# Attention scores and state pass on four 64x64 quarters of the matrix array, in a linear-attention and mixture kernel

## The reference, cut to what matters

```python
# attention: batch 8, heads 8, sequence 576, head width 64, all fp32
scores = scale * np.matmul(q, k.transpose(0, 1, 3, 2))
gamma = 1.0 - 2.0 ** (-5.0 - np.arange(H, dtype=np.float32))
Dmat = np.where(rel >= 0, gamma[:, None, None] ** rel[None, :, :], 0.0)
ret = scores * Dmat[None, :, :, :]
x = np.matmul(ret, v)
...
# then, on 4608 tokens x 512: a soft mixture of 8 experts with 32 slots, and
# a, b = x @ w1, x @ w2 ; out = (a * b) @ w3 @ w_out
```

## Time and profile before

| what | value |
|---|---|
| median of 3 runs (lowest, highest) | 434.02 us (432.9, 434.08) |
| the profiled execution's own time | 434.21 us |
| its span, first to last instruction | 432.4 us |
| granted TensorE clock, mean | 0.995 of 2.4 GHz |
| PE busy | 402.9 us, 93% |
| DVE, ACT, POOL busy | 172.8, 137.3, 165.4 us |
| bytes moved by DMA | 103.57 MB, 240 GB/s on average |

### The profile page before, as it was taken

The page is one execution under the profiler, slowest core; times in us unless marked ns, Lnnn a source line. Parts: engine busy times, 40 slices in busy tenths (PEclk is TensorE's granted clock), DMA queues, the critical chain, the costliest instruction groups (busy, mean ns, idle before and its releaser), DMA issues.

```text
span 432.4 us, 8735 instructions
## 1 busy us (share of the span) xinstructions
PE 402.9 (93%) x3375; PEld 298.1 (69%) x3375; DVE 172.8 (40%) x276; ACT 137.3 (32%) x278; POOL 165.4 (38%) x154
## 2 busy tenths in 40 slices
PE   2899998999999999899999999959989999998897
PEld 2888686878688778746454544448768888787775
DVE  1444364545454545335003100289852344423550
ACT  0224222232233223342233321413254444323442
POOL 2212212122111221074444442078865366544560
PEclk9999999999999999999999999989999999999999
DMA  7986979799969898988979999042222444344432
GB/s 251 314 296 223 332 272 386 236 306 305 385 234 314 306 344 278 343 278 258 330 227 342 386 387 405 7 91 100 93 93 103 171 174 157 116 172 172 172 124 97
DMA packets 50551, 103.57 MB, mean 240 GB/s; under 512 B 4128, under 2 KB 8416, under 8 KB 50528
## 3 DMA queue, kind: packets, MB, share of 16 engines
q1 hardware_dynamic: 50528, 103.26, 68.3%
HBM read 92.92 MB, written 10.32 MB: 239 GB/s over the span
## 4 chain that ended last, share of the span: by engine, by line
PE 73%; DMA 12%; DVE 4%; POOL 3%; SPq 3%; issue 3%; ACT 2%; ACTq 0%; DVEq 0%; POOLq 0%
PE psum L948 14%; PE psum L762 12%; PE psum L618 8%; PE psum L645 8%; PE psum L777 7%; PE psum L635 7%; DMA c_sb<-c_rows 6%; DMA pkg_sb<-in_tiles 5%; PE psum L684 4%; PE psum L916 4%; PE psum L670 3%; PE psum L719 3%; PE psum L695 2%; SPq L510 2%; POOL feat L590 2%
## 5 line engine op out<-in xcount | busy, mean ns | idle before, releaser
L546 POOL TENSOR_TENSOR pkg_sb<-pkg_sb,const_sb 128x512 f32<-128x512 f32 x36 | 37.5, 1042 | 137.8 <-DMA pkg_sb<-in_tiles 137.8
L590 POOL TENSOR_TENSOR feat<-c_sb 128x512 f32<-128x512 f32 x45 | 62.6, 1413 | 45.7 <-DMA c_sb<-c_rows 29.5
L1136 DVE TENSOR_TENSOR weights_t<-psum,const_sb 128x512 f32<-128x512 f32 x72 | 49.2, 690 | 74.2 <-PE psum L645 40.1
L948 PE MATMUL psum<-m_hi,feat_hi 128*128 128x512 f32 x144 | 56.6, 393 | 5.0 <-ACT out_sb L1117 3.4
L948 PE MATMUL psum<-m_hi,feat_lo 128*128 128x512 f32 x144 | 56.1, 390 | 0.0
L948 PE MATMUL psum<-m_lo,feat_hi 128*128 128x512 f32 x144 | 56.0, 389 | 0.0
L618 PE MATMUL psum<-pkg_sb 64*128 64x128 f32 x576 | 43.7, 293 | 11.6 <-DMA pkg_sb<-in_tiles 11.4
L394 DVE TENSOR_TENSOR feat_lo<-feat,feat_hi 128x512 fp32r<-128x512 f32 x32 | 28.4, 888 | 60.3 <-ACT feat_hi L1085 58.3
L618 PEld LDWEIGHTS psum<-pkg_sb 64*128 64x128 f32 x576 | 36.7, 195 | 18.1 <-issue 13.6
L969 ACT COPY state_sb<-psum 64x256 f32<-64x256 f32 x64 | 23.5, 367 | 80.1 <-PE psum L670 79.3
L1085 ACT CAST feat_hi<-feat 128x512 fp32r<-128x512 f32 x45 | 27.7, 624 | 55.6 <-POOL feat L590 55.6
(11 more groups left out here) (126 smaller groups left out, 540.3 us busy)
## 6 DMA issues: line engine op xcount, KB each, us to landing
pkg_sb<-in_tiles SPq DMA_DIRECT2D x72, 256.0 KB, 5.7
pkg_sb<-in_tiles SPq DMA_DIRECT2D x36, 512.0 KB, 5.6
unit_a<-in_moe_w SPq DMA_DIRECT2D x10, 1024.0 KB, 8.3
c_sb<-c_rows SPq DMA_DIRECT2D x36, 256.0 KB
out<-out_sb SPq DMA_DIRECT2D x36, 256.0 KB, 7.0
unit_a<-in_moe_w SPq DMA_DIRECT2D x14, 512.0 KB, 6.9
fold_raw<-in_moe_fold SPq DMA_DIRECT2D x12, 512.0 KB, 7.2
unit_x<-in_moe_w SPq DMA_DIRECT2D x6, 1024.0 KB, 6.8
```

Source lines behind the costliest of these rows:

```text
L546: nc.gpsimd.tensor_tensor(v_nat(t).rearrange("p (h d) -> p h d", h=HEADS), v_nat(t).rearrange("p (h d) -> p h d", h=HEADS), decay.unsqueez ...
L590: nc.gpsimd.tensor_tensor(feat[:, k, :], c_sb[:, s, x, :], c_sb[:, s, y, :], ALU.mult).then_inc(feat_ready, 1)
L948: last = mm(psum[:, OUT + b, :], x, y, start=(at == 0 and m == 0), stop=(at == 4 and m == 2))
L1136: tt(weights_t[:, u % 3, :].rearrange("p (i n) -> p i n", i=4), psum[:, u % 3, :].rearrange("p (i n) -> p i n", i=4), const_sb[:, m:m + P] ...
```

## The change

The attention's layout changes; what is computed stays the same, except that a quarter of the scores, which the mask would set to zero, isn't computed.

- Scores: each head's multiplication is cut in two by keys. One half of the keys (64) goes to PSUM partitions 0 to 63, the other to 64 to 127, so that with even and odd heads on the two halves of the input partitions there are four 64x64 quarters of the array. In the half with the later keys only the later 64 queries are computed, 64 columns in place of 128. For heads 4 to 7 the halves are swapped (the host swaps k and v and the masks too). 16 multiplications for a tile in place of 8. Even heads write bank 0, odd heads bank 1; with two banks in place of three, `scores` waits for both masks of the tile before it.
- State pass: 8 multiplications 64x64 against 128 queries in place of 4 with 128x128; `state_sb` holds states alone, without zeros, and ACT copies it in one instruction of 128 partitions x 256. It is issued right behind `scores`, ahead of the first transposes and of `through_scores`, in tile 4 too.
- Outputs lie in two banks, one for even and one for odd heads, half a bank each.
- The masked scores have four buffers in place of three; both masks of a tile wait for the outputs of the tile two before it.
- In tile 4 the state is summed over all 128 partitions; POOL sets the first half of k to zero (one more instruction of 128x512 for a group).
- The mask constants grow by 256 columns and two more are added: `const_sb` gets 0.13 MB more.
- The loops over groups 1 to 3 are written out on every engine.

```diff
-        OUT_T, STATE, X_NAT, LOGITS, MISC = 3, 4, 5, 6, 7
+        OUT_T, STATE, X_NAT, LOGITS, MISC = 2, 4, 5, 6, 7
...
             def scale_v(g, t):
                 pool.wait_ge(natural_loaded[t % 3], (g * 3 + (t // 3 + 1)) * 16)
+                if t == SEAM:
+
+                    k = k_nat(t).rearrange("p (b n) -> p b n", b=2)
+                    second = const_sb[:, C_SEAM:C_SEAM + 2].unsqueeze(2).to_broadcast([P, 2, D // 2])
+                    nc.gpsimd.tensor_tensor(k, k, second, ALU.mult)
...
-                    pe.wait_ge(masked, g * (2 * TILES) + (2 * t - 1))
+                first = is_first(g) and t == 0
+                if not first:
+
+                    pe.wait_ge(masked, g * (2 * TILES) + 2 * t)
                 for a in range(PAIRS):
                     for odd in range(2):
-                        last = mm(psum[:, (2 * t + odd) % 3, P * a:P * (a + 1)], k_t(t)[HD * odd:HD * (odd + 1), a, :],
-                                  q_t(t)[HD * odd:HD * (odd + 1), a, :], start=True, stop=True)
...
+                        rows = slice(HD * odd, HD * (odd + 1))
+                        for half in range(2):
+
+                            later = half == (0 if a >= 2 else 1)
+                            lo = HD if later and not first else 0
+                            last = mm(psum[HD * half:HD * (half + 1), odd, P * a + lo:P * (a + 1)],
+                                      k_t(t)[rows, a, HD * half:HD * (half + 1)], q_t(t)[rows, a, lo:P],
+                                      start=True, stop=True)
+                            if a == PAIRS - 1:
+                                last.then_inc(scores_ready[odd], 1)
...
+            def through_state(g, t):
+
+
+                pe.wait_ge(x_t_ready, g * TILES + t)
+                pe.wait_ge(state_copied, g * STATES + t)
+                n = P // 2 if t == SEAM else P
+                for a in range(PAIRS):
+                    for odd in range(2):
+                        rows = slice(HD * odd, HD * (odd + 1))
+                        mm(out_of(a, odd, n), state_sb[rows, (t - 1) % 2, a, :], q_t(t)[rows, a, 0:n],
+                           start=(a < 2), stop=True, skip_group_check=True)
...
                 for t in range(TILES):
                     if t < TILES - 1:
                         scores(g, t + 1)
+                    if t > 0:
+                        through_state(g, t)
                     for turned in TURNS[t][:-1]:
                         turn_x(g, turned)
-                    outputs(g, t)
+                    through_scores(g, t)
...
-            with pe.Fori(1, GROUPS) as g:
+            for g in range(1, GROUPS):
                 group(g)
...
-                for r in (0, HD):
-                    copy(state_sb[r:r + HD, t % 2, :, r:r + HD], bank[r:r + HD, :, :]).then_inc(state_copied, 1)
+                copy(state_sb[:, t % 2, :, :].rearrange("p a n -> p (a n)"),
+                     psum[:, STATE, 0:PAIRS * HD]).then_inc(state_copied, 1)
...
-                    if not (is_first(g) and u < 3):
-
-                        dve.wait_ge(out_ready, g * TILES + (t - 1 + hf))
+                    if not (is_first(g) and t < 2):
+
+                        dve.wait_ge(out_ready, g * TILES + (t - 1))
```

More of the change, by code:

```diff
@@ L224, in build @@
         natural_loaded = [sem(f"natural_loaded{i}") for i in range(3)]
[L225 removed]
         v_ready = sem("v_ready")
[L227 removed]
+        scores_ready = [sem(f"scores_ready{i}") for i in range(2)]
         masked = sem("masked")
@@ new lines, in through_scores @@
+            def through_scores(g, t):
+                if t == 0 and not is_first(g):
+                    pe.wait_ge(x_t_ready, g * TILES)
+                pe.wait_ge(masked, g * (2 * TILES) + (2 * t + 2))
+                pe.wait_ge(v_ready, g * TILES + (t + 1))
+                for half in range(2):
+                    for odd in range(2):
+                        for a in (2 * half, 2 * half + 1):
+                            h = 2 * a + odd
+                            last = mm(out_of(a, odd), v_nat(t)[:, HD * h:HD * (h + 1)],
+                                      weights_t[:, (2 * t + odd) % 4, P * a:P * (a + 1)],
+                                      start=(t == 0 and a < 2), stop=True, skip_group_check=True)
@@ L851, in _ @@
             for k in range(4):
-                last = mm(psum[:, MISC, SLOTS * k:SLOTS * (k + 1)], group_sum[:, 0, P * k:P * (k + 1)], fold_rows,
-                          start=True, stop=True)
+                for odd in range(2):
+                    at = HD * PAIRS * odd + HD * k
+                    last = mm(psum[HD * odd:HD * (odd + 1), MISC, SLOTS * k:SLOTS * (k + 1)],
+                              group_sum[:, 0, at:at + HD], fold_rows, start=True, stop=True)
             last.then_inc(slot_in_turned, 1)
@@ L1009, in group @@
                         exp_combine(g - 1)
-            act.wait_ge(state_zeroed, 1)
             group(0)
-            with act.Fori(1, GROUPS) as g:
+            for g in range(1, GROUPS):
                 group(g)
@@ L1200, in _ @@
             group(0)
-            with dve.Fori(1, GROUPS) as g:
+            for g in range(1, GROUPS):
                 group(g)
```

111 lines of the change are left out of this document (48 added, 63 removed).

## The result

The changed kernel takes 424.25 us (median of 4 runs, 421.86 to 425.01) against 433.85 for the kernel before beside it (4 runs, 432.9 to 434.08): a ratio of 0.9772, 95% interval 0.9747 to 0.9798. The gain is 9.6 us; 21.7 were forecast. The profiled execution of the changed kernel took 424.09, its span is 422.3 and its clock 0.987.

A forecast was written before the change was run, and what follows sets the result against it. Attention was taken as TensorE-bound with the DMA queue close behind. Groups 1 to 3 save 3 x (7.7 - 2.5) = 15.6 us, group 0 6.1, together 21.7: 434.21 to 412.5 us, own range 408 to 416, whole range 404 to 422.

The forecast's parts named there:

- (a): Scores: four quarters run at once, each at its own pace, 0.68 us of passes; 0.88 kept as a rival.
- lock step: Rival, chance 0.27: each set of four score passes waits for its longest, left-out quarter worth no time; 417.5 us.
- (b): State pass: 16 passes on four quarters, 0.44 us in place of 0.88, one change of array shape gone.
- only two quarters at a time: Rival, chance 0.07: scores and state pass run only two quarters at once; slower, 440 us.
- (c): Tiles 4 and 5: cheaper seam state pass and tile 5 scores and state pass, less one shape change; 1.9 us saved.
- (d): Tile 8, without scores: shorter state pass and the 0.41 us wait for x_t gone; 0.8 us saved.
- (e): Tile 0: two score blocks alone, 0.25 us saved on each, 0.5 together.
- (f): Group 0: ACT's table load runs ahead, so the first state pass starts at about 16.1, not 17.40; 1.2 us saved.
- (g): Costed at nothing: single state copy, masks, score and output banks, POOL's extra multiplication, written-out loops, small multiplications after the attention.
- the queue's share: Gain lost to DMA waits for q: 2.5 of 7.7 us a group in groups 1 to 3, 2.3 in group 0.
- The queue takes more: Rival, chance 0.13: requests stay at 302 to 317 GB/s, groups last 43 us as now; 422 us.

The follow-up runs named there:

- e10: The kernel before, with the 12 requests for first-unit weights issued behind the last tile's; 431.77 us.
- e7: The changed kernel with all 24 requests for fold and first-unit weights of groups 1 to 3 issued after the last tile's; 438.25 us.
- e4: The changed kernel computing all four score quarters, the masked-out one too; 425.67 us.
- e1: The changed kernel with PE's groups 1 to 3 as a loop again, waits hung on added two-column matmuls (11 a group); 422.53 us.
- e11: The same PE instructions as e1, two-column matmuls too, with groups 1 to 3 written out; 427.04 us.
- e2: The kernel before with PE's groups 1 to 3 written out, nothing else; 434.31 us.
- e13: e1 with the 12 requests for first-unit weights issued behind the last tile's; 415.21 us.
- e3: e1 with the loops of ScalarE, VectorE and GpSimd restored too; 423.47 us.
- e12: e1 with half of the output columns left out in seven tiles of nine, all bytes in place; 424.73 us.
- e9: The changed kernel, written out, with the 12 requests for first-unit weights issued behind the last tile's; 417.49 us.
- e6: The same PE instructions as e5, with groups 1 to 3 written out; 428.21 us.
- e5: The changed kernel with PE's groups 1 to 3 as a loop, waits hung on needed matmuls, one in each state pass 128 partitions wide; 425.65 us.

## Why the prediction was wrong, step by step

**What held.** Tile times of a group with little queue pressure, each from the outputs of the tile before to its own, worked out from the timelines of e10 (group 2) and e7 (the shorter of groups 1 and 2), and beside them the change as it was made (group 2):

| tile | 0 | 1 | 2 | 3 | 4 | 5 | 6 | 7 | 8 | sum |
|---|---|---|---|---|---|---|---|---|---|---|
| e10, kernel before | 7.10 | 3.66 | 4.32 | 3.67 | 6.45 | 5.83 | 4.26 | 4.25 | 3.65 | 43.2 |
| e7, change | 6.63 | 2.97 | 3.43 | 2.79 | 6.47 | 4.02 | 3.38 | 3.37 | 2.80 | 35.9 |
| change as made | 6.64 | 4.21 | 6.99 | 3.67 | 6.47 | 4.02 | 4.96 | 3.38 | 2.77 | 43.1 |

PE's own time fell by 7.3 us a group, 7.7 were forecast. (a) The scores go at their own pace: 0.72 to the state pass against 0.73, and e4 gave the 0.92 of the rival. So *lock step* fell. The Trainium skill, TensorE: Matmul & The Clock Gate, Part 3, The mechanism, which has MATMULs start and end in program order, speaks for 0.92 here; the trace does not agree, and in the rows of 100.39 to 100.77 above passes of the state pass start ahead of the last of the scores. (b) State pass 0.58 against 0.54; so *only two quarters at a time* fell too. The ordinary tiles 2, 3, 6 and 7 gained 0.88 each (0.91 forecast), tile 1 0.69, (c) tiles 4 and 5 1.8 (1.9), (d) tile 8 0.85 (0.8), its wait for x_t gone, (e) tile 0 0.47 (0.5). (f) The table load: 1.2 forecast; the state pass started at 15.94 for 16.1. Of (g), the copy, the banks and GpSimd's extra work cost nothing, the masks one wait of 0.7 us in groups 1 to 3. Group 0 gained 5.3 of 6.1.

**The steps that failed** are two; the three groups gained 4.5 us in place of 15.6. The first is in (g): "the written-out loops (the tile in the earlier trace rows is already written out, and PE works through it without a gap)", costed at nothing. The earlier trace rows are one tile of group 0 in which the DMA engines were 0.62 busy (window 37 to 42). In groups 1 to 3 the change passes through 19 packets, one for each 6.7 us, while requests take 6 us to land. That is 8.4 us of pauses, 7.6 of them behind a packet, and two falls of the clock of 1.7 each: 11.8 us in groups 1 to 3. I had looked at what instructions cost an engine, not at the fact that they come through the same 16 DMA engines. Not all of it is lost for that reason alone: with the same PE work, the loop gives 4.5 us in the median (e1 against e11). The rest goes to the queue at once, and that is the second step, the queue's share, put at 2.5 us a group.

The Trainium skill, Runtime: NRT & Kernel Launch, Instruction fetch mechanics, says that the refill at each 16 KiB costs one tail-bump, "mostly hidden", and that kernels prefer full unrolling. In e2 the trace agrees (0.2 us of pauses in groups 1 to 3, with 13 packets); in the changed kernel it does not: six pauses of 0.6 to 1.9 us behind 19 packets.

**The queue's share** was too small. The forecast, 7.7 less 2.5, asks for groups of some 39 us. No run with all bytes in the stretch came below 40.6, with packets or without. e1's groups of 40.7 do stand only 2.4 above the same PE's pace of 38.3, which e13 shows in group 2; but e3's, with the same PE list, stand 3.7 to 4.9 above it, that PE is 2.4 us slower than the change's own, and in e12 PE's shorter work brought nothing. Against the change's own pace of 35.9 the queue takes 4.8 us a group or more. And moving half of the extra bytes away gives 6.8 us (e9) or 7.3 (e13 against e1), more than the loop's 4.5. *The queue takes more*, at 422, came nearest in time and names half of the cause: the groups run at 317 to 331 GB/s, 41.6 to 43.1 us for 13.6 MB, near the 43 that it said. Its other half was the packets, which no rival had. With both brakes off, the change is the difference between e10 and e13, 16.6 us, and e13 still carries some 7 us of two-column matmuls. So PE's work alone is worth 23 to 24 us by this estimate. That is near the forecast's 21.7 by luck: 21.7 is what was left after 9.8 us had been taken off for the queue.

**What stays open.** When a packet is asked for cannot be read from the trace, only when it passes, so why e2's 13 packets between 50 and 181 us (one for 10 us) cost nothing and the change's 19 cost 8.4 is argued from the spacing against the 6 to 8 us of a landing, not shown. Spacing alone does not settle it: e6 and the change have the same 19 packets in groups of nearly the same length, with 1.5 and 8.4 us of pauses. e11's spread leaves 1 to 2 us of its difference uncertain, e9's more: its runs reach from 5 us below e13's median to 4 above. A loop without any extra matmul was not tried, so what the queue takes from the change's own PE work without packets is not measured.

## What to carry to other kernels

A step costed at nothing needs its cover at the busiest place, not where it happens to be visible: the written-out loop cost nothing in the kernel before (e2) and some 4.5 us in the changed one, whose PE comes to a packet each 6.7 us in place of 10, with the queues fuller. Before shortening an engine's work, find what its time would be with the next limit alone (move the bytes away, e7, or thin out its work, e12): here they show 36.5 us a group without the extra bytes, and no kernel below 40.6 in a stretch that moves 13.6 MB. And here the cure was to move bytes from a full stretch to one with room behind it, which was worth three times as much after the change as before.

## What the runs showed of the hardware that I had not expected

- TensorE's instructions pass in packets of 16 KB through the same DMA engines as the data: 32 packets with PE's list written out, 20 in e1 with its loop. In e1 none passed between 92.5 and 166 us, groups 2 and 3: a body of some 6.3 packets (19 for three groups written out) ran twice more without being fetched again.
- In the changed kernel a pause of 1.7 to 1.9 us in the middle of dense work went twice with 3.4 us at 1.2 GHz, and in e9 once one of 2.55; but one of 2.23 in e7 and one of 1.84 in e9 were followed by no such stretch. In e12, whose waits for tiles reach 3.5 us, the groups' mean clock was 0.92 to 0.96.
- One two-column matmul between two blocks on quarters costs 0.26 us of the stream, and in e5 and e6, where one matmul of each state pass has another width and the waits stand ahead of the last state matmul, the tile is 0.57 longer (3.95 for 3.38).
